# Tokens by rows: block transposes on VectorE in place of transposes on TensorE, in a fused layer of gated attention, spectral mixing and a convolutional feed-forward

## The chip, the cores and the metric

The kernel runs on one core of a Trainium2 chip. The metric is the device time of one execution in microseconds, taken as the median of three runs; lower is better.

## The reference

Three blocks follow each other, all in fp32, with 4 batches of 768 tokens and 384 channels (8 heads of 48):

```python
# attention: a state of 48 x 48 for each head, decayed by alpha
state = alpha[t][:, None] * state + outer(k[t], v[t]);  x[t] = q[t] @ state
# mixing
theta = x @ w_theta
y = w_tok_r @ (x * cos(theta)) + w_tok_i @ (x * sin(theta))     # over tokens
u = x + y
u = u + maximum(u @ w_ch, 0)
# feed-forward, 1024 wide, with a convolution of 3 taps over tokens
h = maximum(u @ w_in, 0)
out = (h * sigmoid(conv3(h))) @ w_out
```

The product x * cos(theta) is needed with tokens on the partitions, since the mixing contracts over tokens. The attention leaves x with channels on the partitions, and the product x @ w_theta takes it in that layout. So x is needed both ways.

## The kernel before, in words

Each engine has its own instruction stream. One function, `program`, is run once for each engine and calls places such as `do.turn(b, s)`; an engine executes what it has registered for a place and skips the others. So the order of work on each engine is the order of the places in `program`. Semaphores (`Tally`) carry the dependencies: `t.done(eng, n)` waits for event n, `t.before(eng, n, back)` waits until the event `back` before n is over, which guards a buffer.

**Attention.** 16 pairs of heads pass through `pair_step`, some 4.8 us each, and the last one through `pair_tail`. The results go to `x_scratch` in DRAM, channels by tokens. Pairs 5 to 12 stay on the chip and are stored in mixing steps 0 to 2 of batch 0 by `store_late`: 12, 8 and 12 DMAs.

**Mixing.** `mix_batch(b)` runs over s = 0 to 5, the six tiles of 128 tokens of a batch; batch 0 is written out, batches 1 and 2 are a hardware loop, batch 3 is written out again. A tile (b, s) is handled in this way, over several steps:
- SyncE loads it, three tiles ahead, into `x_in` (`load`, L754): 128 channels by 3 by 128 tokens, runs of 512 B.
- ScalarE rounds it into `x_t[0]` (`halve`, L979), and VectorE makes the rest, `x_t[1]` (`lower`, L1166). With such pairs three matmul passes give an fp32 product (`PASSES`).
- TensorE turns it into `x_bank` in PSUM with three transposes (`turn`, L1450), and ScalarE copies it to `x_tokens` (`hold`, L985).
- TensorE computes theta with nine matmuls (`theta`, L1462). VectorE brings it into the sine's range with five instructions (`angle`, L1172 to L1184), ScalarE computes sine and cosine (`sines`, L991 to L994), VectorE multiplies both with `x_tokens` (`product`, L1192), and ScalarE and VectorE split the products into pairs `z` (`round_z`, L1001 and L1198). VectorE also copies the tile to `x_all` (L1207).
- TensorE mixes it with 72 / 2 = 36 matmuls over all 768 tokens (`mix`, L1475).

In step s TensorE computes theta of tile s+1, turns tile s+2 and mixes tile s. In the last step of a batch it mixes first; VectorE and ScalarE then form the sums u (`sums`, L1234, L1028, L1240), and two halves of the channel product follow (`end`, L1505).

**Weights in batch 0.** The token weights come in 12 pieces of 384 KB (two for a tile: w_tok_i, w_tok_r), the channel weights as piece 12. SyncE loads them with `refill_piece` (L701): pieces 4 to 7 in step 0, 8 and 9 in step 2, 10 and 11 in step 3, 12 in step 4. ScalarE rounds each one (`high`, L952) and VectorE makes the rest (`low`, L1215). On ScalarE pieces 2s+3 and 2s+4 stand at the end of step s, so piece 10 stands in step 3, ahead of `halve(1, 0)` and `sines(0, 5)` of step 4. A tile's mixing needs both of its pieces.

On SyncE a step is: `load`, then weight pieces, then late stores, all in one queue. `store` in `pair_tail` sends the last two pairs (L734) ahead of tile (0,3).

**Feed-forward.** 64 steps, each of nine matmuls up (L1521) and nine down (L1534), from about 317 us to the end.

Of the kernel before, what the change touches and what calls it, by code (L numbers as in the profile page):

```python
# [22 lines left out]
HALF = SEQ // 2  # L23
HALO = 1
WIDE = HALF + 2 * HALO
PI = 3.14159274
# [196 lines left out]
PLACES = """refill_piece score scan_after scale_k spread cap by_token inside scan_before scale_q mask mask_late select added  # L223
scan_state high bring keep low theta_high theta_low compare waves refill refill_v judge place divert decide store store_half store_late halve hold turn lower theta angle sines
product round_z fill load load_first load_weight spare prepare mix sums end send join front gate split back_ff fetch""".split()
Work = namedtuple("Work", PLACES, defaults=[nothing] * len(PLACES))
# [4 lines left out]
def program(eng, do):  # L231
# [7 lines left out]
    def pair_step(i):  # L239
        p, o = i - 1, i - 2  # L240
        do.scan_after(i)
        if o >= 0:
            do.scan_state(o)
        do.scale_k(i)
        do.spread(i)
        if i <= JUDGED_AT:
            do.cap(i)
        do.scan_before(i)
        do.scale_q(i)
        if p == JUDGED_AT:  # L250
# [12 lines left out]
        if o >= 0:  # L263
            do.inside(o, 1)
        if p >= 0:
            do.added(p)
        for n in compared_in(i):
            do.compare(n)
        if i == JUDGED_AT - 1:
            do.cap(LAST_PAIR)  # L270
        if i == LAST_PAIR:
            do.theta_high()
        if o >= 0:
            for half in range(2):
                do.bring(o, half)
                do.keep(o, half)
        do.refill(i)
        for n in range(KEPT_LATE[0]):
            for half in range(2):
                if i == STORED_FROM + 2 * n + half:  # L280
                    do.store_half(n, half)
        do.refill_v(i)
        if i == JUDGED_AT:
            do.refill_piece(0)
            do.decide()
            do.load_first(0)
            do.refill_piece(1)
            do.load_first(1)
            do.load_first(2)
        if o > KEPT_LATE[-1]:  # L290
            do.store(o)

    def pair_tail():
# [31 lines left out]
        do.angle(0, 0)  # L325
# [20 lines left out]
    def mix_batch(b, last=False):  # L346
        for s in range(T):
            tile(do.load, b, s + 3, last)
            if s == T - 1:
                do.mix(b, s)  # L350
                do.sums(b)
            tile(do.halve, b, s + 2, last)
            tile(do.hold, b, s + 2, last)
            if not (isinstance(b, int) and b == 0 and s == 0):
                tile(do.theta, b, s + 1, last)
            tile(do.angle, b, s + 1, last)
            tile(do.sines, b, s + 1, last)
            tile(do.turn, b, s + 2, last)
            tile(do.lower, b, s + 2, last)
# [65 lines left out]
def layer(nc, ctx, a_rows, k_rows, q_rows, v_rows, v_tokens, w_theta, w_tok_r, w_tok_i, w_ch, w_in, taps_in, w_out,  # L425
# [175 lines left out]
    x_got = [tally(f"x_got{i}", 16) for i in range(3)]  # L601
    x_turned, theta_made, mixed = tally("x_turned", 1, 3), tally("theta_made", 1, 1), tally("mixed", 2, 2)
    x_high, x_low, x_moved, x_kept = tally("x_high"), tally("x_low", 1, 3), tally("x_moved", 1, 1), tally("x_kept", 1, 3)
    turned_by, whole, first, second, bounded = (tally(x, 1, 1) for x in ("turned", "whole", "first", "second", "bounded"))
# [84 lines left out]
    def _(sp):  # L689
# [143 lines left out]
        for t in stored:  # L833
            t.open(sp)
        sp.sem_inc(c_got[0].sem, 16)
        program(sp, Work(refill_piece=refill_piece, refill=refill, refill_v=refill_v, decide=decide, store=store, store_half=store_half, store_late=store_late, load_first=load_first,
                         load=load, load_weight=load_weight, spare=spare, prepare=prepare, end=store_u, back_ff=back_ff))
        stored[0].done(sp, BATCH - 1)
# [70 lines left out]
    def _(act):  # L909
# [70 lines left out]

        def hold(b, s):
            n = b * T + s
            x_turned.done(act, n)
            z_done.before(act, n, 2)
            act.activation(x_tokens[s % 2][:, :], x_bank[:, 0:MODEL], ACT.Copy).then_inc(x_moved.sem, 1)  # L985

        def sines(b, s):
# [85 lines left out]
        act.activation(unused[:, :], state_decay[0][:, 0, ENTERED:], ACT.Copy)  # L1073
        for t in (x_moved, sized, sined, cosined, z_high, *u_stored, c_high, h_done, gate_done, g_high, evacuated):
            t.open(act)
# [3 lines left out]
        program(act, Work(by_token=by_token, mask_late=mask_late, keep=keep, spread=spread, cap=cap, high=high, theta_high=theta_high, compare=compare, waves=waves,  # L1079
                          halve=halve, hold=hold, sines=sines, round_z=round_z, load_weight=load_weight, spare=spare,  # L1080
                          prepare=prepare, sums=sums_of, send=send, fetch=fetch, front=front, gate=gating, split=split, back_ff=back_ff))

    @block.vector
    def _(dve):
# [35 lines left out]
        def scan_before(i):  # L1120
# [6 lines left out]
            if i == 1:  # L1127
                for t in (x_low, turned_by, whole, first, second, bounded, z_done, x_kept, u_done, out_done,
                          c_low, conv1_done, conv2_done, conv3_done, gated_done, z_low, g_low, in_low):
                    t.open(dve)  # L1130
# [37 lines left out]
        def angles(b, s):  # L1168
# [130 lines left out]
        for u in range(3):  # L1299
# [7 lines left out]
        program(dve, Work(scan_after=scan_after, scan_before=scan_before, place=place, mask=mask, scan_state=scan_state,  # L1307
                          divert=divert, lower=lower, angle=angles, fill=fill, product=product, theta_low=theta_low, low=low, round_z=round_z, load_weight=load_weight, sums=sums_of, end=end, spare=spare,
                          prepare=prepare, fetch=fetch, front=front, gate=gating, split=split))

    @block.tensor
    def _(pe):
# [129 lines left out]

        def turn(b, s):
            n = b * T + s
            x_got[s % 3].done(pe, b * (T // 3) + s // 3)
            x_moved.before(pe, n, 1)
            if isinstance(b, int) and b == 0 and s == 0:
                before_done.done(pe, LAST_PAIR)
            for d in range(MODEL_TILES):
                ins = pe.transpose(x_bank[:, d * P:(d + 1) * P], x_in[s % 3][:, d, :], ident[:, :])  # L1450
            ins.then_inc(x_turned.sem, 1)

        def theta(b, s):
# [56 lines left out]
        def join():  # L1510
            x_moved.done(pe, LAST_TILE)
            first.done(pe, LAST_TILE)
# [24 lines left out]

        for t in (x_turned, theta_made, mixed, multiplied, h_made, added_up):
# [7 lines left out]
        program(pe, Work(inside=inside, bring=bring, added=added, judge=judge, score=score, divert=divert, turn=turn, theta=theta,  # L1546
                         mix=mix, end=end, join=join, front=front, back_ff=back_ff))


# [52 lines left out]
```

## Time and profile before

| | |
|---|---|
| Runs | 531.76, 532.25, 532.94 us; median 532.25 us |
| Span of the profiled execution | 530.5 us; the median of the runs is 1.75 us above it |
| TensorE busy | 522.1 us (98%) |
| VectorE busy | 441.2 us (83%) |
| ScalarE busy | 287.4 us (54%) |
| GpSimd busy | 72.0 us (14%) |
| DMA | 56.93 MB, 107 GB/s over the span |

The profile shows one execution. Its span runs from the first to the last instruction; no other time of that execution is recorded, so a sum is made against the span, and the difference to the runs' median is what lies around it. Busy time of TensorE counts overlapping matmuls once. SPq and ACTq are the instruction queues of SyncE and ScalarE; a DMA's row there is the time that its issue took, not its transfer.

### The profile page before, as it was taken

The page shows a single profiled execution, that of the slowest core. Times are in us where ns is not written, and L with a number is a line of the kernel's source. Part 1 is how long each engine was busy: PE and PEld are TensorE (multiplying, and loading weights), DVE is VectorE, ACT ScalarE, POOL GpSimd, SP SyncE. Part 2 cuts the span into 40 slices and gives each one's busy share as a digit, 9 for nine tenths or more (in the row PEclk, how much of TensorE's full clock was granted, in tenths as well). Part 3 has the DMA queues.
Part 4 walks back from the last instruction along what each step waited for, and adds up shares of the span by engine and source line. Part 5 has one row for each costly group of instructions (what it writes and reads, how often), then busy time and mean ns, then how long its engine had stood idle before and what let it go on. Part 6 is the DMA issues. An engine that isn't in the chain of part 4 may idle for free.

```text
span 530.5 us, 11806 instructions
## 1 busy us (share of the span) xinstructions
PE 522.1 (98%) x4142; PEld 513.2 (97%) x4142; DVE 441.2 (83%) x801; ACT 287.4 (54%) x607; POOL 72.0 (14%) x65
## 2 busy tenths in 40 slices
PE   8999999999999999999999999999999999999997
PEld 7999988999999999999999999999999999999997
DVE  8999996997886759767786777999888888889874
ACT  4889887765534434444344542555555454545353
POOL 5988893000000000000000000000000000000000
PEclk9999999999999999999999999999999999999999
DMA  8999987476131020211062011202020110201011
GB/s 326 336 308 361 313 302 224 120 236 222 40 104 31 17 70 25 96 30 54 15 205 94 1 45 56 80 2 90 0 89 30 59 56 33 89 0 47 0 46 44
DMA packets 37163, 56.93 MB, mean 107 GB/s; under 512 B 3328, under 2 KB 27392, under 8 KB 37120
## 3 DMA queue, kind: packets, MB, share of 16 engines
q1 hardware_dynamic: 34000, 51.65, 29.3%
q10 hardware_dynamic: 3120, 4.72, 2.5%
q8 instruction: 26, 0.43, 0.3%
q14 instruction: 17, 0.14, 0.1%
HBM read 42.20 MB, written 14.16 MB: 106 GB/s over the span
## 4 chain that ended last, share of the span: by engine, by line
PE 92%; SPq 2%; DVE 2%; DMA 2%; issue 1%; ACT 0%; POOL 0%; DVEq 0%; ACTq 0%
PE y_bank L1475 26%; PE y_bank L1534 19%; PE theta_bank L1521 10%; PE x_bank L1521 10%; PE y_bank L1505 7%; PE theta_bank L1462 7%; PE weighed L1372 4%; PE x_sum L1330 3%; PE x_sum L1345 2%; PE turned L1357 2%; SPq L734 1%; PE x_bank L1450 1%; DMA x_in<-x_scratch 1%; PE turned L1377 1%; PE x_sum L1316 1%
## 5 line engine op out<-in xcount | busy, mean ns | idle before, releaser
L1534 PE MATMUL y_bank<-first_w,z 128*128 128x384 f32 x576 | 109.5, 335 | 0.0
L1534 PEld LDWEIGHTS y_bank<-first_w,z 128*128 128x128 f32 x576 | 101.2, 188 | 0.0
L1475 PE MATMUL y_bank<-first_w,z 128*128 128x384 f32 x432 | 78.0, 337 | 0.1
L1475 PE MATMUL y_bank<-rest_w,z 128*128 128x384 f32 x432 | 76.9, 336 | 0.0
L1475 PEld LDWEIGHTS y_bank<-first_w,z 128*128 128x128 f32 x432 | 74.5, 188 | 0.3 <-issue 0.3
L1475 PEld LDWEIGHTS y_bank<-rest_w,z 128*128 128x128 f32 x432 | 74.7, 188 | 0.0
L1045 ACT ACTIVATE out_rows<-theta_bank 128x386 f32<-128x386 f32 x32 | 15.8, 493 | 50.6 <-PE theta_bank L1521 50.5
L1275 DVE TENSOR_SCALAR x_rows<-out_rows,taps 128x384 f32<-128x384 f32 x64 | 26.8, 419 | 19.5 <-ACT out_rows L1045 19.4
L1462 PE MATMUL theta_bank<-theta_w,x_t 128*128 128x384 f32 x216 | 41.6, 336 | 0.1
L1278 DVE SCALAR_TENSOR_TENSOR x_rows<-out_rows,taps,x_rows 128x384 f32<-128x384 f32 x64 | 39.6, 619 | 2.3
L1282 DVE SCALAR_TENSOR_TENSOR z_full<-out_rows,taps,x_rows 128x384 f32<-128x384 f32 x64 | 39.6, 619 | 2.2
L1505 PE MATMUL y_bank<-u_part,channel_w 128*128 128x384 f32 x216 | 38.7, 336 | 0.0
L1462 PEld LDWEIGHTS theta_bank<-theta_w,x_t 128*128 128x128 f32 x216 | 37.7, 188 | 0.3 <-DVE x_t L1166 0.3
L1505 PEld LDWEIGHTS y_bank<-u_part,channel_w 128*128 128x128 f32 x216 | 37.3, 188 | 0.2 <-DVE u_part L1240 0.2
L1045 ACT ACTIVATE out_rows<-x_bank 128x386 f32<-128x386 f32 x32 | 15.7, 491 | 39.8 <-PE x_bank L1521 39.8
L979 ACT ACTIVATE x_t<-x_in 128x384 fp32r<-128x384 f32 x24 | 12.6, 523 | 44.9 <-PE theta_bank L1462 36.1
L1295 DVE TENSOR_TENSOR z<-x_tokens,z 128x384 fp32r<-128x384 f32 x64 | 35.3, 552 | 1.3 <-ACT z L1057 1.2
L1521 PE MATMUL theta_bank<-rest_w,in_w 128*128 128x386 f32 x176 | 36.2, 338 | 0.0
L1521 PE MATMUL x_bank<-rest_w,in_w 128*128 128x386 f32 x176 | 36.2, 338 | 0.0
L1057 ACT ACTIVATE z<-x_tokens 128x384 fp32r<-128x384 f32 x64 | 33.1, 517 | 4.8 <-DVE x_tokens L1290 4.3
L991 ACT ACTIVATE sine<-angle 128x384 f32<-128x384 f32 x24 | 12.6, 526 | 42.5 <-DVE angle L1184 42.5
L1372 PE MATMUL weighed<-q_scaled,k_scaled 64*128 64x128 f32 x384 | 31.7, 283 | 1.8 <-POOL q_scaled L855 0.9
(126 smaller groups left out, 974.9 us busy)
## 6 DMA issues: line engine op xcount, KB each, us to landing
a_in<-in_a_rows SPq DMA_DIRECT2D x15, 390.0 KB, 5.8
k_in<-in_k_rows SPq DMA_DIRECT2D x15, 384.0 KB, 5.7
q_in<-in_q_rows SPq DMA_DIRECT2D x14, 384.0 KB, 5.3
v_in<-in_v_tokens SPq DMA_DIRECT2D x16, 288.0 KB, 4.8
x_in<-x_scratch SPq DMA_DIRECT2D x24, 192.0 KB, 2.5
y<-x_all SPq DMA_DIRECT2D x7, 576.0 KB, 3.2
u_scratch<-u_sum ACTq DMA_DIRECT2D x6, 576.0 KB, 3.5
u_first<-u_scratch SPq DMA_DIRECT2D x4, 577.5 KB, 4.4
```

The lines of the kernel that those rows point to most:

```text
L1045: act.activation(h[k % 4], h_bank[k % 2][:, 0:WIDE], ACT.Relu).then_inc(h_done.sem, 1)
L1057: act.activation(g[k % 4][0][:, :], gated[k % 2], ACT.Copy).then_inc(g_high.sem, 1)
L1275: dve.tensor_scalar(conv1[i], h[k % 4][:, 0:HALF], taps[:, 0, f:f + 1], None, ALU.mult).then_inc(conv1_done.sem, 1)
L1278: dve.scalar_tensor_tensor(conv2[i], h[k % 4][:, HALO:HALO + HALF], taps[:, 1, f:f + 1], conv1[i], ALU.mult, ALU.add).then_inc(conv2_done. ...
L1282: dve.scalar_tensor_tensor(conv3[i], h[k % 4][:, 2 * HALO:WIDE], taps[:, 2, f:f + 1], conv2[i], ALU.mult, ALU.add).then_inc(conv3_done.sem, 1)
L1295: dve.tensor_tensor(g[k % 4][1][:, :], gated[k % 2], g[k % 4][0][:, :].bitcast(F32), ALU.subtract).then_inc(g_low.sem, 1)
L1372: return pe.matmul(weighed[:, BLOCKS_OF.index((g, c)), :], k_scaled[p % 2][half_of(g), tokens_of(c)], q_scaled[p % 3][half_of(g), tokens_o ...
L1462: ins = pe.matmul(theta_bank[:, 0:MODEL], x_t[xp][:, d, :], theta_w[wp][:, d, :], start=i == 0 and d == 0, stop=i == 2 and d == MODEL_TILE ...
L1475: ins = pe.matmul(y_bank[2 * d + half][:, 0:HALF], z[s % 2][part][zp][:, d * P:(d + 1) * P], mixing_w(part, wp, s)[:, half_tokens(half)], ...
L1505: ins = pe.matmul(y_bank[2 * d + half][:, 0:HALF], channel_w[wp][:, c, d * P:(d + 1) * P], u_part[up][:, c, half_tokens(half)], start=i == ...
L1521: ins = pe.matmul(h_bank[k % 2][:, 0:WIDE], in_w[wp][:, d, f * P:(f + 1) * P], u_c[half][up][d], start=i == 0 and d == 0, stop=i == 2 and ...
L1534: ins = pe.matmul(out_bank[half][t][:, 0:MODEL], g[k % 4][gp][:, t * P:(t + 1) * P], out_w[wp][f], start=f == 0 and i == 0, stop=f == FF_T ...
```

## The change

The tokens-on-partitions form of x no longer comes from TensorE. VectorE's `transpose` turns each block of 32 by 32 within a tile by itself. So that a whole tile comes out right, the tile is loaded a second time, as `x_blocks`: partition t * 32 + p holds, for each n, the 32 tokens of block t of channel n * 32 + p. That takes four DMAs a tile, one for each group of 32 partitions, each of 32 x 12 runs of 32 tokens (128 B). One VectorE instruction, `flip`, then writes `x_tokens`.

`load_blocks` stands on SyncE right behind `load`, three tiles ahead; for the first three tiles it stands in the pair step of pair 14 and in `pair_tail`. `flip(b, s+1)` stands first among VectorE's work of a step. `turn` (TensorE) and `hold` (ScalarE) go.

```diff
         if i == JUDGED_AT:
             do.refill_piece(0)
             do.decide()
             do.load_first(0)
             do.refill_piece(1)
             do.load_first(1)
             do.load_first(2)
+            do.load_blocks(0, 0)
+            do.load_blocks(0, 1)
...
         for n in range(SPLIT_EARLY, LOADED_EARLY):
             do.refill_piece(n)
+        do.load_blocks(0, 2)
...
         do.store(o)
-        do.turn(0, 0)
         do.lower(0, 0)
         do.theta_low()
         do.theta(0, 0)
-        do.turn(0, 1)
         do.scan_state(p)
         do.low(0)
-        do.hold(0, 0)
+        do.flip(0, 0)
         do.high(1)
         do.halve(0, 1)
-        do.hold(0, 1)
         do.angle(0, 0)
...
         for s in range(T):
             tile(do.load, b, s + 3, last)
+            tile(do.load_blocks, b, s + 3, last)
+            tile(do.flip, b, s + 1, last)
             if s == T - 1:
                 do.mix(b, s)
                 do.sums(b)
             tile(do.halve, b, s + 2, last)
-            tile(do.hold, b, s + 2, last)
             if not (isinstance(b, int) and b == 0 and s == 0):
                 tile(do.theta, b, s + 1, last)
             tile(do.angle, b, s + 1, last)
             tile(do.sines, b, s + 1, last)
-            tile(do.turn, b, s + 2, last)
             tile(do.lower, b, s + 2, last)
...
+    x_blocks = ring("x_blocks", 3, [P, MODEL // BLOCK, BLOCK])
...
-            for t in (x_turned, x_low, x_kept):
+            for t in (x_low, x_kept):
                 t.before(sp, b * T + s, 3)
             load_tile(b, s)
+
+        def load_blocks(b, s):
+            x_flipped.before(sp, b * T + s, 3)
+            for t in range(P // BLOCK):
+                sp.dma_start(x_blocks[s % 3][t * BLOCK:(t + 1) * BLOCK, :, :],
+                             x_scratch.rearrange("b (n p) t -> b p n t", p=BLOCK)[b, :, :, s * P + t * BLOCK:s * P + (t + 1) * BLOCK]
+                             ).then_inc(blocks_got[s % 3].sem, 16)
...
+        def flip(b, s):
+            n = b * T + s
+            blocks_got[s % 3].done(dve, b * (T // 3) + s // 3)
+            z_done.before(dve, n, 2)
+            dve.transpose(x_tokens[s % 2][:, :], x_blocks[s % 3][:, :, :].rearrange("p n t -> p (n t)")).then_inc(x_flipped.sem, 1)
+
         def product(b, s):
             n = b * T + s
             z_low.before(dve, n, 1)
-            x_moved.done(dve, n)
+            x_flipped.done(dve, n)
...
         def join():
-            x_moved.done(pe, LAST_TILE)
             first.done(pe, LAST_TILE)
...
-    nc = bacc.Bacc("TRN2", target_bir_lowering=False, num_devices=1)
+    nc = bacc.Bacc("TRN2", target_bir_lowering=False, num_devices=1, dynamic_dma_scratch_size=1024)
```

## Rows read from the trace of the kernel before

**Rows 1.** The page: busy time, and the chain's shares.

```profile
PE 522.1 (98%) x4142; PEld 513.2 (97%) x4142; DVE 441.2 (83%) x801; ACT 287.4 (54%) x607; POOL 72.0 (14%) x65
...
PE 92%; SPq 2%; DVE 2%; DMA 2%; issue 1%; ACT 0%; POOL 0%; DVEq 0%; ACTq 0%
```

**Rows 2.** The chain, two mixing steps: start us, us, what.

```profile
161.63 1.56 PE theta_bank L1462 x9
163.52 6.24 PE y_bank L1475 x36
169.76 1.56 PE theta_bank L1462 x9
```

**Rows 3.** Timeline of VectorE in an ordinary step: start us, us, engine line.

```profile
229.72 0.56 DVE L1172 TENSOR_SCALAR turns<-theta_bank 128x384 f32<-128x384 f32 x1 [1.80 <-PE theta_bank L1462]
```

**Rows 4.** Timeline of SyncE's issues, 72 to 160 us.

```profile
100.15 0.41 SPq L754 DMA_DIRECT2D x_in<-x_scratch  x1
...
110.28 0.41 SPq L754 DMA_DIRECT2D x_in<-x_scratch  x1
...
116.46 6.55 SPq L734 DMA_DIRECT2D x_scratch<-x_late  x12
...
123.67 0.48 SPq L701 DMA_DIRECT2D out_rows<-in_moe_w_tok_i  x1
```

**Rows 5.** Timeline, 100 to 160 us, and the chain: TensorE around two mixings.

```profile
112.86 0.55 PE L1450 MATMUL x_bank<-ident,x_in 128*128 128x128 f32 x3 [0.89 <-DMA x_in<-x_scratch]
...
113.40 6.25 PE y_bank L1475 x36
...
129.70 12.49 PE y_bank L1475 x72
```

**Rows 6.** Timeline of VectorE and ScalarE, 126 to 136 us.

```profile
126.53 1.57 ACT L952 ACTIVATE rest_w<-out_rows 128x768 fp32r<-128x768 f32 x2
...
129.41 0.56 DVE L1172 TENSOR_SCALAR turns<-theta_bank 128x384 f32<-128x384 f32 x1 [0.81 <-PE theta_bank L1462]
...
131.98 0.53 ACT L991 ACTIVATE sine<-angle 128x384 f32<-128x384 f32 x1 [1.61 <-DVE angle L1184]
...
134.68 1.03 DVE L1198 TENSOR_TENSOR z<-z_full,z 128x384 fp32r<-128x384 f32 x2 [0.46 <-ACT z L1001]
```

**Rows 7.** The page: DMA issues, KB each, median us to landing.

```profile
out_rows<-in_moe_w_tok_i SPq DMA_DIRECT2D x4, 384.0 KB, 3.7
```

**Rows 8.** Groups by line: busy us, mean ns of one.

```profile
L1207 DVE COPY x_all<-x_in 128x384 f32<-128x384 f32 x24 | 13.1, 546 | 0.1
...
L1174 DVE TENSOR_SCALAR turns<-turns 128x384 f32<-128x384 f32 x24 | 8.6, 360 | 0.8
```

**Rows 9.** The tile x_in: ns min/median/max, and its DMAs' landing.

```profile
L754 SPq DMA_DIRECT2D x_in<-x_scratch x24: 367/373/488, 82.3 to 286.2; - x24
...
DMA to landing us min/median/max: 2.4/2.5/4.6
```

**Rows 10.** Timeline, 186 to 216 us, at the end of batch 1.

```profile
200.42 1.49 DVE L1240 TENSOR_TENSOR u_part<-u_sum,u_part 128x384 fp32r<-128x384 f32 x3
...
202.10 9.63 PE L1505 MATMUL y_bank<-u_part,channel_w 128*128 128x384 f32 x54
```

**Rows 11.** Windows (DMA share and GB/s last), and ScalarE's DMA queue.

```profile
161.00:164.00 3.00, 3.00 (x20) 2.97 (x19) 1.34 (x4) 0.72 (x2) 0.00 (x0) 1.00 0.26 71
...
84.00:88.00 4.00, 3.60 (x80) 3.21 (x78) 2.89 (x4) 3.19 (x5) 0.38 (x1) 1.00 1.05 300
100.00:136.00 36.00, 35.11 (x207) 34.69 (x207) 31.76 (x60) 23.17 (x43) 0.00 (x0) 1.00 0.69 216
...
q10 hardware_dynamic: 3120, 4.72, 2.5%
```

**Rows 12.** Groups by line: the same matmul form at the start and later.

```profile
L1543 PE MATMUL weighed<-x_tokens 128*128 128x128 f32 x26 | 4.9, 372 | 1.8 <-DVE x_tokens L1297 1.8
...
L1316 PE MATMUL x_sum<-x_tokens 128*128 128x128 f32 x26 | 3.7, 287 | 0.0
```

More of the change, by code:

```diff
@@ L24 @@
 HALO = 1
+BLOCK = 32
 WIDE = HALF + 2 * HALO
@@ L223 @@
 PLACES = """refill_piece score scan_after scale_k spread cap by_token inside scan_before scale_q mask mask_late select added
-scan_state high bring keep low theta_high theta_low compare waves refill refill_v judge place divert decide store store_half store_late halve hold turn lower theta angle sines
-product round_z fill load load_first load_weight spare prepare mix sums end send join front gate split back_ff fetch""".split()
+scan_state high bring keep low theta_high theta_low compare waves refill refill_v judge place divert decide store store_half store_late halve flip lower theta angle sines
+product round_z fill load load_first load_blocks load_weight spare prepare mix sums end send join front gate split back_ff fetch""".split()
 Work = namedtuple("Work", PLACES, defaults=[nothing] * len(PLACES))
@@ L601, in layer @@
     x_got = [tally(f"x_got{i}", 16) for i in range(3)]
-    x_turned, theta_made, mixed = tally("x_turned", 1, 3), tally("theta_made", 1, 1), tally("mixed", 2, 2)
-    x_high, x_low, x_moved, x_kept = tally("x_high"), tally("x_low", 1, 3), tally("x_moved", 1, 1), tally("x_kept", 1, 3)
+    blocks_got = [tally(f"blocks_got{i}", 16 * (P // BLOCK)) for i in range(3)]
+    theta_made, mixed = tally("theta_made", 1, 1), tally("mixed", 2, 2)
+    x_high, x_low, x_flipped, x_kept = tally("x_high"), tally("x_low", 1, 3), tally("x_flipped", 1, 3), tally("x_kept", 1, 3)
     turned_by, whole, first, second, bounded = (tally(x, 1, 1) for x in ("turned", "whole", "first", "second", "bounded"))
@@ L836, in _ @@
         program(sp, Work(refill_piece=refill_piece, refill=refill, refill_v=refill_v, decide=decide, store=store, store_half=store_half, store_late=store_late, load_first=load_first,
[L837 removed]
+                         load_blocks=load_blocks, load=load, load_weight=load_weight, spare=spare, prepare=prepare, end=store_u, back_ff=back_ff))
         stored[0].done(sp, BATCH - 1)
@@ L979, in halve @@
             act.activation(x_t[0][:, :, :], x_in[s % 3][:, :, :], ACT.Copy).then_inc(x_high.sem, 1)
[L981 to L985, printed above, removed]
         def sines(b, s):
@@ L1073, in _ @@
         act.activation(unused[:, :], state_decay[0][:, 0, ENTERED:], ACT.Copy)
-        for t in (x_moved, sized, sined, cosined, z_high, *u_stored, c_high, h_done, gate_done, g_high, evacuated):
+        for t in (sized, sined, cosined, z_high, *u_stored, c_high, h_done, gate_done, g_high, evacuated):
             t.open(act)
@@ L1079, in _ @@
         program(act, Work(by_token=by_token, mask_late=mask_late, keep=keep, spread=spread, cap=cap, high=high, theta_high=theta_high, compare=compare, waves=waves,
-                          halve=halve, hold=hold, sines=sines, round_z=round_z, load_weight=load_weight, spare=spare,
+                          halve=halve, sines=sines, round_z=round_z, load_weight=load_weight, spare=spare,
                           prepare=prepare, sums=sums_of, send=send, fetch=fetch, front=front, gate=gating, split=split, back_ff=back_ff))
@@ L1127, in scan_before @@
             if i == 1:
-                for t in (x_low, turned_by, whole, first, second, bounded, z_done, x_kept, u_done, out_done,
+                for t in (x_low, x_flipped, turned_by, whole, first, second, bounded, z_done, x_kept, u_done, out_done,
                           c_low, conv1_done, conv2_done, conv3_done, gated_done, z_low, g_low, in_low):
@@ L1307, in _ @@
         program(dve, Work(scan_after=scan_after, scan_before=scan_before, place=place, mask=mask, scan_state=scan_state,
-                          divert=divert, lower=lower, angle=angles, fill=fill, product=product, theta_low=theta_low, low=low, round_z=round_z, load_weight=load_weight, sums=sums_of, end=end, spare=spare,
+                          divert=divert, lower=lower, flip=flip, angle=angles, fill=fill, product=product, theta_low=theta_low, low=low, round_z=round_z, load_weight=load_weight, sums=sums_of, end=end, spare=spare,
                           prepare=prepare, fetch=fetch, front=front, gate=gating, split=split))
@@ L1441, in divert @@
             by_state.if_out_of_range(pe, in_range, by_state.path_tensor)
[L1443 to L1451, printed above, removed]
         def theta(b, s):
@@ L1536, in back_ff @@
                 ins.then_inc(added_up.sem, 1)
-        for t in (x_turned, theta_made, mixed, multiplied, h_made, added_up):
+        for t in (theta_made, mixed, multiplied, h_made, added_up):
             t.open(pe)
@@ L1545, in _ @@
         pe.wait_ge(dve_const, N_DVE_CONST)
-        program(pe, Work(inside=inside, bring=bring, added=added, judge=judge, score=score, divert=divert, turn=turn, theta=theta,
+        program(pe, Work(inside=inside, bring=bring, added=added, judge=judge, score=score, divert=divert, theta=theta,
                          mix=mix, end=end, join=join, front=front, back_ff=back_ff))
```

## The prediction

> **What bounds the kernel now.** First the shares [rows 1]: TensorE is busy for 98% of the span, and the chain that ended last lies on it for 92%; the granted clock is 1.00 in the windows [rows 11]. So time removed from TensorE is a gain unless a new wait takes its place. Then the chain through two ordinary mixing steps [rows 2]: theta's nine matmuls, a hole, 36 mixing matmuls, and theta again. The hole (163.52 less 161.63 + 1.56) is 0.33 us, and in it lie the three transposes into x_bank, the group that stands at 112.86 in another step [rows 5]. In such a step VectorE waits 1.80 us for theta [rows 3], so it isn't the bound.
>
> Batch 0's mixing, from about 96 to 144 us, is another matter. SyncE issues there without a pause from 100.15 until past 123.67: x tiles, weight pieces and 32 late stores [rows 4]. TensorE once waits for what came late: at 112.86 for the x tile issued at 110.28 [rows 5]. And ScalarE's two roundings that begin at 126.53 take pieces 9 and 10; piece 10, issued at 123.67, is taken at about 127.36, 3.7 us after its issue, which is the median landing time of such a piece [rows 4, 6, 7]. SyncE has nothing to spare in this stretch; that decides the case.
>
> **What is removed.** 24 x 3 transposes. On the path they are 0.33 us a tile, 7.9 us in all. The tile wait at 112.86 also leaves TensorE: theta ended at about 111.83 and mixing began at 113.40, so 1.57 us of hole closes, 1.2 us more than the transposes. If nothing new came up, the change would be worth 7.9 + 1.2 = 9.1 us. ScalarE loses 24 copies of half a microsecond; it isn't on the path in these stretches, so they are worth nothing.
>
> **What VectorE gets.** 24 block transposes of 128x384 f32. No row shows one. From below: the single-source TENSOR_SCALAR in SBUF, 360 ns; from above, at ordinary rates, the COPY of a same-sized tile, 546 ns [rows 8]. I take 0.50 us, near the copy, as data is moved and not computed. In batches 1 to 3 it lies in the 1.80 us wait ahead of the angle and costs nothing. In batch 0 that wait is 0.81 us in the step at 129.41 [rows 6] and the period shrinks by 0.33, so 0.5 just fits; 0.1 us more or less moves the sum by 0.2.
>
> **What SyncE gets.** Each tile brings four more DMAs, 96 in all, in SyncE's queue ahead of whatever follows. Bounds for one issue: 0.37 us (the shortest x_in row) and 0.55 us (a late store with its register work, 6.55 us for 12) [rows 4, 9]. The longest x_in row is 0.49 us; behind other DMAs I take 0.45 us, so 1.8 us a tile. In batches 1 to 3 a step of 8 us has room for it. In batch 0, tiles (0,3), (0,4), (0,5) and (1,0) stand ahead of piece 10: 16 issues, 7.2 us, less 0.2 us, since the run of issues starts that much earlier (theta(0,0) no longer stands behind transposes; most of its 0.48 us goes to flip(0,0)). Followed through:
> - Piece 10 is issued at 123.67 + 7.0 = 130.7 and lands 3.7 later, at 134.4.
> - ScalarE stands at its rounding, behind which wait halve(1,0) and sines(0,5), and behind them VectorE's lower, low(10) and product. Rounding 0.8 (two take 1.57) and halving 0.5 give sines at 135.8, where it was 131.98. From there to the first rounded z was 135.23 less 131.98 = 3.25 us [rows 6], so z for tile (0,5) is there at 139.0.
> - TensorE needs it for mix(0,5), which followed mix(0,4) at once, at 129.70 + 6.25 = 135.95 [rows 5]. It now starts at 139.0: +3.05 us, although TensorE is there at about 135. Everything gained so far, the 1.2 included, is lost in this wait.
> - VectorE is late by then too (low(11), low(12), the in_w subtraction, flip(1,0), all ahead of the sums): the channel matmuls of batch 0 start 3.2 us late.
>
> **The rest of the gain.** After that 16 transposed tiles remain: 16 x 0.33 = 5.3 us. At the batch ends the transposes now cover the wait for the last u_part: VectorE ends it at 201.91 (three from 200.42), TensorE's product starts at 202.10 [rows 10], and without the transposes TensorE is ready at about 201.8. I take off 0.2 us for each of two such ends. Net: +3.2 - 5.3 + 0.4 = -1.7 us.
>
> **The transfers.** A tile's blocks are 4 x 384 runs of 128 B, and 64 packets of semaphore. One x_in tile, 400 packets of mostly 512 B, filled 0.26 of 16 queues for 3 us [rows 11]: 12.5 us / 400 = 31 ns a packet. ScalarE's queue shows 2.5% x 16 x 530.5 / 3120 = 68 ns at 1513 B. The line through both gives 18 ns at 128 B. I take 24 ns, 0.6 us of all 16 queues per DMA, 2.4 us a tile: in an ordinary step of 8 us the queues have the room, in batch 0 they go from 0.69 to nearly full. The first blocks meet full queues (84 to 88 us, share 1.05): x tiles (0,1) and (0,2), 0.8 us each, fill them to about 86.4, the blocks take 2.4, and 1.0 passes to the landing (my share of a lone x_in's 2.5 us, of which 0.8 is transfer [rows 9]). So flip(0,0) starts at 89.8, with VectorE free at 89.53. At 18 ns the sum is 1.1 us better; at 31 ns it is 2.2 us worse (0.7 at the first flip, which the chain carries to the store and the x loads, the rest in later landings).
>
> The Trainium skill, DMA: Bandwidth & Descriptors, section Specifications, asks for at least 512 B per transfer and says that below it the DMA engine does a read-modify-write. By that rule a 128 B packet would be no cheaper than one of 512 B; by it the sum would be +0.5 us or worse instead of -1.7. The trace has no 128 B run to settle it.
>
> **Nothing for the rest.** The wider bound on scratch for DMA touches no queue used here: all issues listed are SyncE's and ScalarE's [rows 7]. join() loses a wait that was long over.
>
> **The sum.** The profiled span is 530.5 us; the runs' median, 532.25, is 1.75 above it, taken as constant. 530.5 - 1.7 = 528.8, plus 1.75: 530.5 us (rounded down). The likeliest case's own range: issue 0.37 gives -1.0, 0.55 gives +1.2; packets -1.1 and +2.2; flip 0.2 each way. Together 528.2 to 534.1.
>
> **Rivals.**
> 1. *Late weights eat part of the gain* (above), 0.48: 530.5.
> 2. *Nothing new on the path*, 0.10: SyncE's issues overlap, or piece 10's delay is absorbed. The full 9.1 less 0.4 to 2: 524.0. Against it: piece 10 is taken the moment it can have landed [rows 4, 6].
> 3. *The small packets are dear*, 0.24: slower. At 40 ns a packet each DMA fills the queues for 1.0 us, a tile 4.0. The batch 0 stretch (100 to 136 us, share 0.69) has 0.31 x 36 = 11 us of free queue time, and six tiles want 24. flip(0,0) waits until 86.4 + 4.0 + 1.0 = 91.4; the store of the last pair and all x loads after it start 1.4 later, piece 10 is issued at 132.1 and lands 5 us on, mix(0,5) is 6.6 late and the channel matmuls 8.4; -4.9 after that leaves +3.5: 535.8. It decides from about 30 ns on, where the sum crosses zero; at 31 ns it is 532.7. For it: the full queues at 84 to 88 us. Against it: the slope between the two rows.
> 4. *TensorE's clock falls in the new wait*, 0.10. TensorE would stand idle for some 3.9 us ahead of mix(0,5); the longest idle time it now has there is 0.9 us [rows 5], and the clock stayed at 1.00, its 2.4 GHz level. What slow matmuls cost the first rows show: the same 128x128 form takes 372 ns in the warm-up at the start and 287 ns later, 30% more in a mean that may hold both levels [rows 12]. On one tile's mixing, 6.25 us, 30 to 50% more is +2 to +3; with 530.5, 533.0. The Trainium skill, TensorE: Matmul & The Clock Gate, section Why this matters for your kernels, warns of idle gaps between matmul bursts, after which the clock is halved; by it the wait would cost those 2 to 3 us, by the traces so far nothing.
> 5. *The block transpose is slow*, 0.08: at 1.3 us VectorE can't hide it in batch 0 (0.8 us free) and delays u-sums: 6 x 0.5 more, +3: 533.5. Batches 1 to 3 still hide it in 1.80 - 0.33.
>
> **Chances.** About 0.2% (1.06 us) is what a measurement of this kernel can tell from none. Case 1 gives 0.36 faster, 0.09 same, 0.03 slower; case 2 0.10 faster; case 3 0.06 same, 0.18 slower; case 4 0.03 faster, 0.03 same, 0.04 slower; case 5 0.01, 0.02, 0.05. Sum: 0.50, 0.20, 0.30. The range for all: 527.0 (leaves out most of case 2) to 535.5 (leaves out the dear half of case 3).
>
> **What the changed profile would show.** Right: mixing follows theta with no hole in ordinary steps (theta to theta 7.8 us, not 8.13); no TensorE idle at 112; SyncE busy without a pause from 100 to about 134; ScalarE's L952 rows waiting for DMA into out_rows by 5 us or more at pieces 8 and 10; TensorE idle 3 to 4 us ahead of the last mixing of batch 0; flips of about 0.5 us inside VectorE's wait for theta. Wrong: pieces 8 and 10 on time (then case 2), flips waiting for x_blocks in ordinary steps (case 3), a granted clock below 1.00 after 139 (case 4), flips over 0.8 us (case 5).

## The result

The changed kernel took 534.87 us (median of 4 runs, 533.39 to 535.61) where the kernel before took 532.46 (4 runs, 531.76 to 532.94): ratio 1.0044, 95% interval [1.0025, 1.0063]. The forecast was 530.5 us, 527.0 to 535.5. It is slower, by 2.4 us, where 1.75 us faster was forecast. The profiled execution is the quickest of the four: 533.39 us, span 531.7 (before: 532.25 and 530.5). One execution further down, act_rest's of 570.6 us at a mean granted clock of 0.85, was in the chip's slow state and is in no median and no ratio.

The page of the changed kernel first: busy time, the granted clock in 40 slices, the chain's shares, and the new DMA group.

```profile
PE 518.2 (97%) x4070; PEld 507.2 (95%) x4070; DVE 452.5 (85%) x825; ACT 278.2 (52%) x583; POOL 72.2 (14%) x65
...
PEclk9999999998999999999999999999999999999999
...
PE 85%; SPq 8%; issue 2%; DVE 2%; DMA 1%; ACT 0%; POOL 0%; DVEq 0%; ACTq 0%
...
x_blocks<-x_scratch SPq DMA_DIRECT2D x96, 48.0 KB, 2.4
```

TensorE is busy for 3.9 us less than before [rows 1], and yet the span is 1.2 us longer. The chain says why: SyncE's queue had 2% of it, now it has 8%, and the clock has a slice below 9.

SyncE's issues around batch 0, the timeline of the changed kernel (start us, us, engine line, count), which answers to [rows 4]:

```profile
84.88 5.59 SPq L778 DMA_DIRECT2D x_blocks<-x_scratch  x8
...
95.72 5.78 SPq L737 DMA_DIRECT2D x_scratch<-x_rows  x8
...
101.60 0.41 SPq L757 DMA_DIRECT2D x_in<-x_scratch  x1
102.07 2.04 SPq L778 DMA_DIRECT2D x_blocks<-x_scratch  x4
...
131.03 0.41 SPq L757 DMA_DIRECT2D x_in<-x_scratch  x1
131.48 2.01 SPq L778 DMA_DIRECT2D x_blocks<-x_scratch  x4
133.54 0.47 SPq L704 DMA_DIRECT2D out_rows<-in_moe_w_tok_i  x1
```

The x tile that was issued at 100.15 goes at 101.60; from there to piece 10 it takes 31.9 us, where it took 23.5. Piece 10 is issued 9.9 us later than before.

The chain from there on (start us, us, what), which answers to [rows 2, 5]:

```profile
133.54 3.49 DMA out_rows<-in_moe_w_tok_i
...
137.81 0.52 ACT x_t L990
...
138.35 0.47 DVE x_t L1171
...
138.82 0.95 DVE rest_w L1226
...
140.89 0.57 DVE z L1209
...
141.59 6.48 PE y_bank L1476 x36
148.07 1.56 PE theta_bank L1463 x9
149.64 9.54 PE y_bank L1506 x54
159.18 1.56 PE theta_bank L1463 x9
160.75 6.45 PE y_bank L1476 x36
167.19 1.56 PE theta_bank L1463 x9
168.75 6.24 PE y_bank L1476 x36
174.99 1.04 PE theta_bank L1463 x6
```

The reader sees both halves of the case. Above: mix(0,5) hangs on piece 10 through ScalarE's halving, VectorE's lower, low(10) and product, and the rounding of z, and starts at 141.59, 5.64 us later than before (135.95); the channel matmuls of batch 0 start at 149.64, 5.56 later (144.08). Below: theta, mixing and theta follow without a hole, 7.80 us from 167.19 to 174.99, where a step took 8.13. From the channel matmuls of batch 0 to the end it is 531.7 - 149.64 = 382.06 us, before 386.42: 4.36 us come back. 5.56 - 4.36 = 1.2 us is the difference of the two spans.

The other three executions of the changed kernel have spans of 532.7 to 533.9 and a mean granted clock of 0.994 to 0.997. Of the 2.4 us between the medians, the two profiled executions show 1.2; the other 1.2 lie in executions of which there is no trace, and stay open.

### The profile page after: what moved, and what is told of

Its sections match the earlier page's. It is cut to its first block, busy times and chain, and to the rows that moved or that the text cites. A ratio compares the mean times of both kernels' runs of the same rounds, so it can differ in the third digit from the quotient of the medians.

```text
span 531.7 us, 11820 instructions
## 1 busy us (share of the span) xinstructions
PE 518.2 (97%) x4070; PEld 507.2 (95%) x4070; DVE 452.5 (85%) x825; ACT 278.2 (52%) x583; POOL 72.2 (14%) x65
## 4 chain that ended last, share of the span: by engine, by line
PE 85%; SPq 8%; issue 2%; DVE 2%; DMA 1%; ACT 0%; POOL 0%; DVEq 0%; ACTq 0%
PE y_bank L1476 22%; PE y_bank L1534 19%; PE theta_bank L1521 10%; PE x_bank L1521 10%; PE y_bank L1506 7%; PE theta_bank L1463 5%; PE weighed L1383 4%; SPq L737 4%; PE x_sum L1341 4%; SPq L778 3%; PE x_sum L1356 2%; PE turned L1368 1%; SPq L704 1%; PE turned L1388 1%; DMA out_rows<-in_moe_w_tok_i 1%
## 5 line engine op out<-in xcount | busy, mean ns | idle before, releaser
L1476 PEld LDWEIGHTS y_bank<-rest_w,z 128*128 128x128 f32 x432 | 75.8, 190 | 4.1 <-issue 4.1
L1286 DVE TENSOR_SCALAR x_rows<-out_rows,taps 128x384 f32<-128x384 f32 x64 | 26.8, 419 | 19.6 <-ACT out_rows L1050 19.5
L990 ACT ACTIVATE x_t<-x_in 128x384 fp32r<-128x384 f32 x24 | 12.5, 521 | 40.0 <-PE theta_bank L1463 31.4
```

The source lines that it names most:

```text
L1286: dve.tensor_scalar(conv1[i], h[k % 4][:, 0:HALF], taps[:, 0, f:f + 1], None, ALU.mult).then_inc(conv1_done.sem, 1)
L1476: ins = pe.matmul(y_bank[2 * d + half][:, 0:HALF], z[s % 2][part][zp][:, d * P:(d + 1) * P], mixing_w(part, wp, s)[:, half_tokens(half)], ...
```

## The experiments

Each row of this table is one kernel: the median, the ratio to the runs of the kernel before beside it (532.2, 532.56 and 532.33 us in three series; the ratio comes from all the runs and isn't the quotient of the two medians), and from its profiled execution the start of piece 10's issue, the time from the issue of x tile (0,1), which stands just ahead of the first block loads, to that of piece 10 ("stretch"), the start of mix(0,5) and of the channel matmuls of batch 0, and the span less this last ("rest").

| kernel | us | ratio, 95% interval | piece 10 | stretch | mix(0,5) | channel | rest |
|---|---|---|---|---|---|---|---|
| before | 532.46 | 1 | 123.67 | 40.28 | 135.95 | 144.08 | 386.42 |
| changed | 534.87 | 1.0044 [1.0025, 1.0063] | 133.54 | 49.67 | 141.59 | 149.64 | 382.06 |
| after_again | 534.16 | 1.0035 [1.0016, 1.0053] | 132.78 | 48.84 | 140.97 | 149.02 | 382.08 |
| no_blocks | 526.3 | 0.9902 [0.9886, 0.9919] | 123.59 | 40.37 | 134.31 | 142.36 | 382.04 |
| one_issue | 529.38 | 0.9948 [0.9930, 0.9967] | 128.42 | 43.68 | 137.24 | 146.88 | 382.02 |
| long_runs | 532.4 | 1.0019 [1.0000, 1.0038] | 131.18 | 47.02 | 139.07 | 148.68 | 382.02 |
| late_blocks | 533.06 | 1.0016 [1.0005, 1.0028] | 131.62 | 48.43 | 140.09 | 149.70 | 382.00 |
| fill | 533.0 | 1.0005 [0.9985, 1.0026] | 137.78 | 49.35 | 146.36 | 154.17 | 381.93 |
| act_rest | 534.63 | 1.0063 [1.0039, 1.0087] | 124.38 | 40.33 | 141.11 | 150.73 | 382.07 |
| turns_kept | 536.7 | 1.0078 [1.0056, 1.0099] | 131.91 | 48.53 | 140.04 | 148.41 | 386.39 |
| hybrid | 527.38 | 0.9910 [0.9892, 0.9928] | 123.25 | 40.05 | no wait | 142.78 | 382.02 |
| hybrid_again | 527.15 | 0.9894 [0.9873, 0.9916] | 123.81 | 40.33 | no wait | 143.41 | 381.99 |

The theory was that SyncE's issues, by their number and not by what they carry, make the weights of batch 0 late. The rivals were the small packets, the place of the issues, and the clock. The stretch sorts the kernels: with no block load in SyncE's queue between tile (0,3) and piece 10 it is 40.05 to 40.37 us, as before; with sixteen of them, in runs of 128 B, it is 48.53 to 49.67.

**No block loads after the first three tiles (no_blocks).**

```diff
         def load_blocks(b, s):
+            if not (isinstance(b, int) and b == 0 and s < 3):
+                return
             x_flipped.before(sp, b * T + s, 3)
...
-            blocks_got[s % 3].done(dve, b * (T // 3) + s // 3)
+            blocks_got[s % 3].done(dve, 0)
```

> Leaves out: the blocks of x are loaded only for the first three tiles, and every later flip turns those again, so y is made from the wrong x in the products. All 24 flips stay, 84 of 96 block DMAs go. Theory S (SyncE's issues push the weight pieces of batch 0 late): pieces 8 and 10 are on time again, the gain of the removed transposes is kept: about 525 us (before less 5 for batches 1 to 3, less 2 for batch 0). Rival V (the flips burden VectorE): nothing changes, about 534.5. Rival P (the 128 B packets fill the queues): about 525 too; the next two runs tell S from P.

Piece 10 is back at 123.59, the clock at 1.0, and the kernel is 1% faster than before. Everything that the change gives (no transposes, the flips on VectorE) is in this kernel; what it is without are the block loads, but for the first twelve. With those twelve in SyncE's queue the stretch is still 40.37 us, so they cost piece 10 nothing here.

From the kernel before to this one the channel matmuls gain 1.72 us: 144.08 - 142.36. Between this one and the changed kernel lie 7.3 us of span, all in batch 0. That is what the loads behind the first three tiles cost.

The flips aren't free in batch 0 all the same. With piece 10 on time, the chain of no_blocks lies on VectorE, and on ScalarE's rounding within its loop, from 96.85 to 134.18, with a flip in each step, and mix(0,5) waits 0.97 us for VectorE's z. Its chain, and its TensorE timeline:

```profile
127.31 0.95 DVE rest_w L1227
128.25 0.49 DVE x_tokens L1196
128.74 0.46 DVE turns L1178
...
134.31 6.48 PE L1477 MATMUL y_bank<-rest_w,z 128*128 128x384 f32 x36 [0.97 <-DVE z L1210]
```

Eight tiles' transposes and the wait at 112 us would give 8 x 0.33 + 1.2 = 3.8 us in batch 0; 1.72 came.

**One DMA for a tile's blocks, with packets as small (one_issue).**

```diff
-            for t in range(P // BLOCK):
...
+            sp.dma_start(x_blocks[s % 3][:, :, :],
+                         x_scratch[b, 0:P, :].rearrange("p (n t) -> p n t", t=2 * BLOCK)[:, :, BLOCK:]
+                         ).then_inc(blocks_got[s % 3].sem, 16)
```

> Leaves out: the blocks' right place; one DMA a tile (instead of four) brings the same 1536 runs of 128 B to the same 128 partitions, but from other rows and tokens of x, so y is wrong. Theory S: a tile costs SyncE 0.5 us and not 2.05, 4 x 1.5 = 6 us less ahead of piece 10: 526 us, and piece 10 issued before 128. Rival P: same packets, same time: 534.5.

Piece 10 comes at 128.42 instead of 133.54. The 4 x 3 issues that are gone behind the first x tile are worth 12 x 0.51 = 6.1 us by the rows above (nine more are gone ahead of it); the stretch is 5.2 to 6.0 us shorter than in the two profiles of the changed kernel. The bytes and the run length are the same, so the number of issues makes most of the delay. Not all of it: four block DMAs are left behind the first x tile, the stretch is 3.4 us above 40.28, and a weight piece issued right behind one takes 0.89 to 0.97 us where it took 0.48 to 0.50. Both expectations, 526 us and piece 10 before 128, were missed, though by less than the rival's 534.5. And mix(0,5) took 8.08 us here, 1.6 more than in the changed kernel:

```profile
137.24 8.08 PE y_bank L1475 x36
145.31 1.56 PE theta_bank L1462 x9
146.88 9.55 PE y_bank L1505 x54
```

The windows of this kernel over those us (busy time by engine; the granted clock, DMA share and GB/s last):

```profile
136.00:140.00 4.00, 2.76 (x12) 2.79 (x13) 3.10 (x6) 3.16 (x5) 0.00 (x0) 0.82 0.68 246
140.00:144.00 4.00, 4.00 (x20) 4.00 (x19) 2.74 (x4) 0.71 (x1) 0.00 (x0) 0.75 0.34 58
```

TensorE had stood for 2.24 us ahead of this mixing. The clock then fell from its 2.4 GHz level for part of it: rival 4 at work, in a kernel whose wait is shorter than the changed kernel's 3.10.

**Four DMAs with runs of 1,536 B (long_runs).**

```diff
-                sp.dma_start(x_blocks[s % 3][t * BLOCK:(t + 1) * BLOCK, :, :],
-                             x_scratch.rearrange("b (n p) t -> b p n t", p=BLOCK)[b, :, :, s * P + t * BLOCK:s * P + (t + 1) * BLOCK]
+                sp.dma_start(x_blocks[s % 3][t * BLOCK:(t + 1) * BLOCK, :, :].rearrange("p n t -> p (n t)"),
+                             x_scratch[b, t * BLOCK:(t + 1) * BLOCK, HALF:SEQ]
```

> Leaves out: the blocks' right place; four DMAs a tile, each 32 runs of 1536 B in place of 384 of 128 B, from other tokens, so y is wrong. Theory S: four issues of some 0.45 to 0.5 us as before: 534 us, piece 10 issued at 132 to 134. Rival P: the small packets are gone: 526.

As many issues, as many bytes, a twelfth of the runs. SyncE's timeline:

```profile
85.17 3.74 SPq L778 DMA_DIRECT2D x_blocks<-x_scratch  x8
...
129.28 1.87 SPq L778 DMA_DIRECT2D x_blocks<-x_scratch  x4
131.18 0.42 SPq L704 DMA_DIRECT2D out_rows<-in_moe_w_tok_i  x1
```

Four issues take 1.87 us instead of 2.01 to 2.04, the first eight 3.74 instead of 5.59. So the form of a DMA costs SyncE some 0.04 us an issue. The stretch is 47.02 us, 1.8 to 2.7 less than in the changed kernel's two profiles, and the ratio 1.0019 where theirs are 1.0035 and 1.0044, with intervals that overlap. That is a part of the loss at most, not its bulk, and how much of it the long runs gave isn't shown: from the first x tile to piece 10 it is 32.01 us, as in the changed kernel (31.94 and 32.30), and ahead of that tile the first eight also took only 4.07 to 4.43 us in no_blocks, turns_kept and after_again, with runs of 128 B.

**The blocks behind the weights and ahead of the late stores in batch 0 (late_blocks).**

```diff
-            tile(do.load_blocks, b, s + 3, last)
+            if not (isinstance(b, int) and b == 0):
+                tile(do.load_blocks, b, s + 3, last)
...
+                tile(do.load_blocks, b, s + 3, last)
                 if s in STORED_LATE:
```

> Only the order on SyncE changes: in batch 0's six steps the four block DMAs stand behind the weight pieces of the step and ahead of the late stores. Piece 8 then has two tiles' blocks ahead of it as before less none, piece 10 three tiles' instead of four: 2 us earlier. Theory S: mix(0,5) 2 us earlier, 532.8 us. Rival P: no change, 534.5.

Twelve block DMAs stand ahead of piece 10 instead of sixteen, worth 2 us, but the stretch is only 0.4 to 1.2 us shorter (48.43), since single block DMAs took 2.04, 1.08 and 0.74 us here. TensorE waited 3.93 us ahead of mix(0,5), which then took 8.05 us at a granted clock of 0.57 in the window 140 to 144: most of that stretch at the 1.2 GHz level. What the place gained, the clock took in this profile. In the changed kernel's own profile the clock fell too, but in mix(0,4), after waits of 1.76 and 0.28 us. Its TensorE timeline:

```profile
128.50 2.36 PE L1463 MATMUL theta_bank<-theta_w,x_t 128*128 128x384 f32 x9 [1.76 <-DVE x_t L1171]
...
131.14 7.35 PE L1476 MATMUL y_bank<-rest_w,z 128*128 128x384 f32 x36 [0.28 <-DVE z L1209]
...
141.59 6.48 PE L1476 MATMUL y_bank<-rest_w,z 128*128 128x384 f32 x36 [3.10 <-DVE z L1209]
```

There it was free, as the wait for z(0,5) followed anyway. Ahead of mix(0,5) it costs 8.05 - 6.48 = 1.57 us on the path.

**The changed kernel once more, and with matmuls in its waits (after_again, fill).** fill puts 8 matmuls that nobody reads ahead of theta(0,5) and 18 ahead of mix(0,5):

```diff
+            if isinstance(b, int) and b == 0 and s == T - 1:
+                keep_busy(8)
...
+            if first_batch and s == T - 1:
+                keep_busy(18)
```

> The changed kernel once more, beside the others of this call: 534.7 us, 0.4% above before.

> The changed kernel, with 8 matmuls of ident (128x128) ahead of theta(0,5) and 18 ahead of mix(0,5) on TensorE, in the waits that it has there, into x_bank, which nobody reads. Theory C (part of the loss is TensorE's clock, which falls to its lower level in the waits of batch 0 and costs 1.6 us in the mixing behind them): granted clock 1.00, mix(0,5) in 6.5 us, and about 533.3 us, 1.4 under the changed kernel beside it. Rival S alone: the clock costs nothing on the path, 534.7.

The clock first. None of the 12 executions of after_again has a mean granted clock above 0.997; of fill's 13, eleven have 0.999 or 1.0. Within after_again five executions with 0.997 have a median of 532.8 us, seven with 0.993 or 0.994 one of 535.6. So with work in the waits the lower mean is mostly gone, and in after_again it goes with the slower executions. That it makes them slow isn't shown: 2.8 us is more than the 1.57 of one mixing, so a late execution may as well be what lets the clock fall; in late_blocks eight executions with 0.997 have a median of 533.3, three with 0.999 or 1.0 one of 532.96; and the mean doesn't say where the clock fell. In time, fill is 1.2 us ahead of after_again (95% interval -0.3 to 3.1, resampled from the runs of both): not settled. Its price is seen in the chain:

```profile
135.84 6.50 PE y_bank L1484 x36
142.35 4.02 PE x_bank L1471 x36
146.36 6.24 PE y_bank L1484 x36
```

The 18 matmuls (36 records) take 4.02 us where the wait was some 3, so about 1 us of what they saved is spent again. This profiled execution (537.85 us) is the longest of fill's 13: its clock was 0.57 from 12 to 16 us and 1.00 from 96 to 148, and its first x tile was already issued 4.7 us later than the changed kernel's (87.44 against 82.75). So its times in the table aren't to be compared with the others', only its stretch and its rest.

**From tile (0,3) on, the block loads in ScalarE's queue (act_rest).** In each step, behind the rounding of z:

```diff
-            tile(do.load_blocks, b, s + 3, last)
...
+            tile(do.load_ahead, b, s + 3, last)
...
+                act.dma_start(x_blocks[s % 3][t * BLOCK:(t + 1) * BLOCK, :, :],
```

> From tile (0,3) on ScalarE issues the four block DMAs, behind its rounding of z, and SyncE none. Theory S: SyncE's weight pieces are on time again; ScalarE, free of the copies, has room for 2 us a step: 526.5 to 528 us, near the run without blocks (526.3). Rival P (packets): they move the same bytes from another queue, 534. Rival A: ScalarE's 2 us put off sines and roundings: above 530, with TensorE waiting in ordinary steps too.

This missed, but it separates the issues from the packets: the same packets move, from another queue, and piece 10 is 0.7 us late (124.38) with a stretch of 40.33. mix(0,5) still starts at 141.11. ScalarE and VectorE, timeline of the step at 113 us:

```profile
112.99 0.32 ACTq L957 DMA_DIRECT2D x_blocks<-x_scratch  x1
...
113.34 1.63 ACTq L957 DMA_DIRECT2D x_blocks<-x_scratch  x3
...
115.02 0.85 ACT L973 ACTIVATE first_w<-out_rows 128x768 fp32r<-128x768 f32 x1 [1.51 <-issue]
...
115.90 0.96 DVE L1239 TENSOR_TENSOR first_w<-out_rows,first_w 128x768 fp32r<-128x768 f32 x1 [1.28 <-ACT first_w L973]
116.78 0.57 DVE L1208 STREAM_TRANSPOSE x_tokens<-x_blocks 128x384 f32<-128x384 f32 x1
```

The four issues hold ScalarE for about 2 us. Behind them stands the rounding of a weight piece, for which VectorE waits 1.28 us with the next flip and the next angle behind it; the angle gives the sines, and the sines the rounded z that stands ahead of the next issues. The loop closes at 9.09 us a step (sines at 110.71, 119.80, 128.88, 137.99), 1.3 over the 7.80 that TensorE needs for theta and mixing, and the queue that was to be relieved is replaced by another. This is what [rows 6] could have told: in batch 0 ScalarE and VectorE wait for each other in both directions.

**The transposes left on TensorE, unread (turns_kept).**

```diff
+            tile(do.turn, b, s + 2, last)
             tile(do.lower, b, s + 2, last)
```

> The changed kernel with TensorE's three transposes of every tile kept in their old place (nobody reads what they write); VectorE still turns x from the blocks, ScalarE's copy is gone. Theory T (what the change gives back behind batch 0 is the time of the transposes on TensorE alone): in batch 0 TensorE waits for weights anyway and absorbs them, so the channel matmuls of batch 0 start at 149.6 to 150.5; behind them everything comes to 386.4, as in the kernel before, and not to 382.0: span 536 to 537, time 538.3 (ratio 1.011). Rival W (the 4.4 us came from waits on the copy by ScalarE or on its order, which is still gone here): behind batch 0 it stays at 382.0: time 534.2 to 535.

This puts back 22 of the 24 tiles: the transposes of (0,0) and (0,1), ahead of the mixing steps, stay out (4136 matmul records, before 4142), which leaves the rest untouched. The rest is 386.39 us, that of the kernel before to 0.03. So the 4.4 us are TensorE's transposes, with the short waits that they covered; rival W is out. The time came out 1.6 us below what was expected, mostly since batch 0 was 1.2 us ahead of the changed kernel's. TensorE did wait for an x tile here, and the clock fell there (0.83 and 0.74 in the windows from 112 to 120): its timeline:

```profile
114.63 0.89 PE L1459 MATMUL x_bank<-ident,x_in 128*128 128x128 f32 x3 [2.75 <-DMA x_in<-x_scratch]
115.17 7.84 PE L1484 MATMUL y_bank<-first_w,z 128*128 128x384 f32 x36
```

**Batch 0 the old way, the rest the new way (hybrid, hybrid_again).** TensorE's transposes and ScalarE's copies stay for batch 0's six tiles; the blocks of batch 1's first tiles are issued at the end of batch 0's steps, behind the weights.

```diff
+            if not (isinstance(b, int) and b == 0):
+                return
...
+                if s >= T - 3:
+                    do.load_blocks(1, s + 3 - T)
```

> Batch 0's six tiles are transposed by TensorE and copied by ScalarE as before; only batches 1 to 3 load blocks and flip, and batch 1's first three tiles load theirs behind the weights and late stores. Theory S: batch 0 keeps its time (channel matmuls at 144), and the 4.4 us that all changed kernels gain behind it stay: 532.3 - 4.4 = 527.9 us. Rival (packets or flips cost time in any step): above 530.

> The hybrid unchanged, once more, since its four times are few: the old way in batch 0, blocks and VectorE behind it. 527.4 (526.5 to 528.3), ratio 0.991, granted clock 1.0, mix(0,5) without a wait. If the first figure was luck: 529 or above.

It beats both kernels, twice: 0.9910 and 0.9894, 9 executions from 526.5 to 528.3 us, clock 0.999 or 1.0 in all. TensorE doesn't wait ahead of mix(0,5).

4.4 us of the gain are the rest, as everywhere. In the first of the two profiles 1.3 more lie in batch 0: two tiles of batch 1 whose transposes are gone (0.66) and a shorter wait for the x tile at 112 us (0.38 instead of 0.89). In the second it is 0.7.

## Why the prediction was wrong

**The mechanism was right, its size was not.** The likeliest case (late weights) is what happened, but the weights came so late that they ate the whole gain and more, and the sign turned. Its stations can be laid side by side. From the issue of piece 10 on each interval was met: landing and taking 3.5 us (3.7 predicted), from there to mix(0,5) 4.54 us (4.6). The wait for the tile at 112 us was gone, the flip of tile (0,0) began at 89.92 (89.8), ordinary steps have no hole, and in them the flip lies in VectorE's wait for theta. One wait wasn't foreseen: TensorE stood 1.76 us ahead of theta(0,5), behind piece 8, which was issued at 122.77 instead of 115.30; on the path it cost nothing, since mix(0,5) waited for piece 10 anyway. The price of the flip, and that of the wait left, in VectorE's timeline:

```profile
167.52 0.57 DVE L1195 STREAM_TRANSPOSE x_tokens<-x_blocks 128x384 f32<-128x384 f32 x1
...
168.89 0.56 DVE L1177 TENSOR_SCALAR turns<-theta_bank 128x384 f32<-128x384 f32 x1 [0.80 <-PE theta_bank L1463]
```

**The step that failed is "What SyncE gets"**, in two terms.
- *The issue.* I took 0.45 us, the duration of a row; from start to start it is 0.51 (four take 2.04, with gaps of 0.04 between them). From the first x tile to piece 10 it is 31.94 us, before 23.52: 8.4 us for 16 issues, not 7.2. That is +1.2. In after_again it is 32.30 and in turns_kept 33.30, so 8.4 to 9.8 us for the sixteen. The range had this term too narrow as well: 0.55 us an issue makes 16 x 0.10 = +1.6, not the +1.2 that stands there.
- *The start of the run of issues.* I had it 0.2 us earlier than before; it was 1.45 later, at 101.60: +1.65 in this execution. Before, SyncE stood there waiting for the stores' data (the same eight issues of x_rows took 10.04 us, in no_blocks 3.92), so I counted it as free. In the changed kernel twelve block DMAs and the stores behind them fill that room, and single issues take far more than 0.5 us. The chain of the changed kernel:

```profile
87.63 0.56 SPq L778
88.24 1.73 SPq L778
90.00 0.47 SPq L778
...
95.72 1.01 SPq L737
98.43 1.58 SPq L737
```

  These three are 2.8 us above 0.5 each. Where they were fewer (turns_kept, first eight in 4.13 us) the x tile went at 98.61. SyncE's queue holds the same up to there in after_again, no_blocks and act_rest, and the tile went at 100.48, 98.26 and 101.61. So this term differs from execution to execution, between -1.9 and +1.5 us against 100.15, while the first term, the price of the sixteen issues, is there in each execution that has them. What makes an issue slow no run here shows; the queues are nearly full there (DMA share 0.97 at 84 to 88 us).

Together +2.85: piece 10 at 133.54, not 130.7. mix(0,5) is 5.64 late instead of 3.05, the channel matmuls 5.56 instead of 3.2.

**"The rest of the gain"** was 0.5 too good: 4.36, not 4.9. The transposes also covered short waits at each batch's end. The first mixing after it takes 6.45 us instead of 6.27 and the channel matmuls 9.54 instead of 9.38, some 0.34 us in each of the batches, where I took off 0.4 in all. A row of the changed kernel's timeline shows one: the first weight load of the mixing waits for VectorE to empty the bank.

```profile
160.66 6.22 PEld L1476 LDWEIGHTS y_bank<-first_w,z 128*128 128x128 f32 x36 [0.23 <-DVE u_sum L1259]
```

So the profiled span is 528.8 + 2.4 + 0.5 = 531.7.

**The clock (rival 4, 0.10)** I had put at +2 to +3 and as a case of its own. It comes along with the late weights, so the wait and the clock that falls behind it belonged into one case, and where it fell ahead of mix(0,5) its price was 1.57 us, a little under the range. In the changed kernel's own profile it cost nothing on the path. The 1.5 us between that profile and the median, 534.87 - 533.39, stay open: of the four executions the two with a mean clock of 0.997 took 533.39 and 535.61 us, the two with 0.994 took 534.42 and 535.32. The Trainium skill, TensorE: Matmul & The Clock Gate, section Why this matters for your kernels, warns of idle gaps between bursts; these traces agree: mixing of 8.04 to 8.08 instead of 6.48 us behind gaps of 2.24 to 3.93 us in four profiles, though in the changed kernel's profile and in after_again's gaps of 3.10 and 2.88 us left mix(0,5) at 6.48. In both the clock had fallen and risen shortly before, in mix(0,4).

**The small packets (rival 3, 0.24)** gave the right sign for a wrong reason. In 168 to 176 us the changed kernel's queues carried one x tile and one tile of blocks. Windows of the changed kernel:

```profile
100.00:136.00 36.00, 33.53 (x181) 32.15 (x181) 30.65 (x58) 16.47 (x30) 0.00 (x0) 0.95 0.69 194
...
168.00:176.00 8.00, 8.00 (x48) 8.00 (x47) 6.03 (x13) 3.02 (x6) 0.00 (x0) 1.00 0.25 51
```

0.25 x 16 x 8 = 32 us of queue time, less the 12.5 of an x tile [rows 11], is 19.5 us for 1,600 packets: an estimate of 12 ns each, half of the 24 I took, and the share over 100 to 136 us is 0.69 as before, not nearly 1. The Trainium skill, DMA: Bandwidth & Descriptors, section Specifications, speaks of a read-modify-write below 512 B; for these reads of 128 B the trace doesn't bear it out, 12 ns against 31 ns for a 512 B packet.

**The slow flip (rival 5, 0.08)** did not come: all 24 take 565 to 572 ns, and the next instruction starts 0.49 us after. **Nothing new on the path (rival 2, 0.10)** did not come even in no_blocks, 526.3 us where it named 524.0: with the weights on time VectorE's loop with the flips is next, and mix(0,5) waits for it. The prediction had written that "0.5 just fits" there.

Left open: what makes single issues take 0.7 to 2.0 us, what decides in which of two waits the clock falls, and what makes the changed kernel's other executions 1.0 to 2.2 us longer than the profiled one.

## What to carry to other kernels

A DMA queue that issues without a pause is an engine on the path: count each new issue from start to start, and ask what a quiet stretch ahead of it was absorbing before you call it free. Where a moved load pays in some stages and hurts in one, do it by stage: here the same edit costs 5.6 us in batch 0 and gives 4.4 behind it, and doing it only there gives 5. A wait of 2 to 4 us put in front of TensorE can cost more than itself, since the next burst may run at the lower clock (four of six profiles here); and a queue that is moved to a busy engine takes that engine's own loop with it.

## What the runs showed of the hardware

- SyncE needs 0.51 us from issue to issue for a DMA of 32 x 12 runs of 128 B, 0.47 for one of 32 runs of 1,536 B; single issues took 0.7 to 2.0 us. ScalarE needs about 0.5 us each, and nothing behind them started meanwhile (four issues from 112.99 to 114.97, the next instruction at 115.02).
- A 128 B packet costs about 12 ns of one queue, a 512 B packet 31 ns: estimates from the DMA share of one window each.
- VectorE's block transpose of 128x384 f32: 569 ns, 0.49 us to the next start.
- The granted clock fell behind waits of 1.76 to 3.93 us of TensorE in a stretch that had been at 1.00, and stayed at 1.00 behind waits of 2.88 and 3.10 us shortly after such a fall; 36 mixing matmuls took 7.29 to 8.08 us behind a fall instead of 6.48.
